# A two-layer fp32 feed-forward chain: the second layer's first product by Strassen's scheme

## The reference

```python
# 1: retention, 4 batches, 8 heads, 768 tokens, head size 64
state = gamma * state + k_t v_t^T;  y_t = scale * q_t state
# 2: first feed-forward, 512 -> 1024 -> 512
h = x @ w_in;  solu = h * softmax(h);  x = layernorm(solu) * g_ln @ w_out
# 3: second feed-forward, 512 -> 2048 -> 512
h = x @ w_in
g = h * np.cos(h)
out = g @ w_out
```

## Time and profile before

| | us |
|---|---|
| median of 3 executions | 1001.17 |
| lowest, highest | 1001.01, 1001.72 |
| span of the profiled execution | 1000.7 |
| PE busy | 961.5 (96%) |
| DVE busy | 714.2 (71%) |
| ACT busy | 430.6 (43%) |
| POOL busy | 259.8 (26%) |

### The profile page before, as it was taken

How to read it: one execution, slowest core, us unless ns; L and a number is a source line. 1 busy time by engine, 2 the same in 40 slices (tenths; PEclk the granted TensorE clock), 3 DMA queues, 4 the chain that set the end, 5 groups by cost and what they waited for, 6 DMA issues and landing times.

```text
span 1000.7 us, 13925 instructions
## 1 busy us (share of the span) xinstructions
PE 961.5 (96%) x4800; PEld 808.4 (81%) x4800; DVE 714.2 (71%) x1133; ACT 430.6 (43%) x786; POOL 259.8 (26%) x237
## 2 busy tenths in 40 slices
PE   2799999999999999999999999999999999999997
PEld 2688788888888888887788888888888888888886
DVE  6988788887888788885896566565665656656564
ACT  4645445445445454444554434333343433333333
POOL 5453454444544534512233002001100200110000
PEclk8899999999999999999999999999999999999999
DMA  7411221311312212032352100010110101001001
GB/s 261 132 63 53 84 76 53 106 52 52 105 52 64 94 52 88 28 95 87 104 168 64 43 1 26 17 42 0 42 42 0 41 0 42 0 0 42 1 1 43
DMA packets 39857, 57.92 MB, mean 58 GB/s; under 512 B 3217, under 2 KB 15505, under 8 KB 39825
## 3 DMA queue, kind: packets, MB, share of 16 engines
q1 hardware_dynamic: 39824, 57.50, 17.9%
HBM read 44.90 MB, written 12.58 MB: 57 GB/s over the span
## 4 chain that ended last, share of the span: by engine, by line
PE 77%; DVE 14%; issue 4%; ACT 3%; DMA 0%; POOL 0%; SPq 0%; DVEq 0%; ACTq 0%; POOLq 0%
PE bank L284 26%; PE bank L286 25%; PE bank L285 25%; DVE p_l L800 4%; DVE z_l L879 2%; DVE nmax L844 2%; ACT z_h L622 2%; DVE p_m L793 1%; DVE x_l L824 1%; PE bank L484 1%; ACT p_h L589 1%; DVE w1o_l L838 1%; DVE w1i_l L833 1%; DVE stats L855 1%; DVE work L849 0%
## 5 line engine op out<-in xcount | busy, mean ns | idle before, releaser
L908 DVE SCALAR_TENSOR_TENSOR red<-turns,bank 128x512 f32<-128x512 int32 x96 | 65.8, 686 | 155.2 <-ACT turns L648 155.2
L284 PE MATMUL bank<-w2o_h,g_h 128*128 128x512 f32 x384 | 149.8, 390 | 1.3 <-DVE g_l L926 1.2
L284 PE MATMUL bank<-y_g,w2i_h 128*128 (+1 forms) x384 | 149.6, 390 | 0.0
L286 PE MATMUL bank<-w2o_h,g_l 128*128 128x512 f32 x384 | 149.4, 389 | 0.0
L286 PE MATMUL bank<-y_g,w2i_l 128*128 (+1 forms) x384 | 149.4, 389 | 0.0
L285 PE MATMUL bank<-y_g,w2i_h 128*128 (+1 forms) x384 | 149.4, 389 | 0.0
L285 PE MATMUL bank<-w2o_l,g_h 128*128 128x512 f32 x384 | 149.4, 389 | 0.0
L648 ACT ACTIVATE turns<-bank 128x512 int32<-128x512 f32 x96 | 57.3, 597 | 202.5 <-PE bank L286 202.5
L714 POOL TENSOR_TENSOR y_g<-y_raw,y_g 128x512 f32 (+1 forms) x24 | 31.9, 1333 | 307.6 <-ACT y_g L643 307.6
L654 ACT ACTIVATE gg<-red 128x512 f32<-128x512 f32 x96 | 60.7, 632 | 91.5 <-DVE red L912 91.5
L284 PEld LDWEIGHTS bank<-w2o_h,g_h 128*128 128x128 f32 x384 | 72.1, 188 | 17.5 <-issue 2.7
(11 more groups left out here) (96 smaller groups left out, 2061.9 us busy)
## 6 DMA issues: line engine op xcount, KB each, us to landing
raw<-kT SPq DMA_DIRECT2D x24, 256.0 KB, 2.6
raw<-qT SPq DMA_DIRECT2D x24, 256.0 KB, 3.0
raw<-kn SPq DMA_DIRECT2D x24, 256.0 KB, 3.6
raw<-vn SPq DMA_DIRECT2D x24, 256.0 KB, 4.1
y_scratch<-work SPq DMA_DIRECT2D x24, 256.0 KB, 4.0
y_raw<-y_scratch SPq DMA_DIRECT2D x6, 1024.0 KB, 5.2
out<-o SPq DMA_DIRECT2D x24, 256.0 KB, 2.2
w_raw<-w_in SPq DMA_DIRECT2D x16, 256.0 KB, 2.8
```

The source lines that it names most:

```text
L284: eng.matmul(dst, ah, bh, start=first and i == 0, stop=False)
L286: m = eng.matmul(dst, al, bh, start=False, stop=last_one and i == n - 1)
L908: dve.scalar_tensor_tensor(red[:, f % 2, :], turns[:, f % 2, :], -TWO_PI_HI, ps_h2[:, f % 4, :], ALU.mult, ALU.add)\
```

## The change

The first half stays but for its tail. In the second half tokens go in 4 superblocks (`NS`) of 768, two halves of 384, and a superblock in 8 periods (`NJ`), each of two feature tiles, j (called LO) and j + 8 (HI). Feature halves, halves of the 512-long contraction and token halves make a 2 by 2 by 2 block product, which Strassen's scheme (in Winograd's form) does with seven products P1, P2, P6, P5, P3, P7, P4 in that order; each is 2 slices of the contraction by 3 matmuls of 384 columns. Their sums are taken so:

- weights: four sums `S1` to `S4` on POOL (`w2_in_sums`), then seven operands of 128 x 256 are split into high (ACT `w2_in_hi`) and low (DVE `w2_in_lo`), 1792 numbers a partition at once, once a period in superblock 0; they are stored to memory (`w2_split`) and loaded from there in superblocks 1 to 3, into a ring of two periods;
- tokens: four sums on POOL (`y_sums`, `y_sum4`), seven operands of 768 numbers split by ACT `y_hi` and DVE `y_lo` at places in period 7 and period 0 (`SPLIT_HI`, `SPLIT_LO`); DVE has the low parts now, POOL had them;
- results: two PSUM banks, `ps_x` and `ps_y2`, in which later products are added onto earlier ones; ACT copies three states (`e_1`, `e_2`, `e_5`) and one result (`c21`) out, DVE makes the three others (`c11`, `c12`, `c22`), 384 columns each.

The gate works on 768 columns, of LO and HI one after the other in the same two queues. Its square goes from DVE to ACT; the factor -2 goes to the copy of the outputs, of which DVE now has every second one. The second products `l4` have 6 token tiles, and stand between the seven products by the table `FILL`: HI of the period before the last, LO of the last. `ps_out` has six banks. Each product waits for the copy that frees its bank (`l3`). In the tail of the first half, P1 to P7 of period 0 replace `L3` 0 to 3.

```diff
-BLK = 512
-NBLK = NTOK // BLK
+HALF = 384
+SUPER = 2 * HALF
+NS = NTOK // SUPER
+NJ = NF // 2
+TS = SUPER // 128
...
+P1, P2, P6, P5, P3, P7, P4 = range(7)
+A21, A11, A12, A22, S1, S2, S3, S4 = range(8)
+WEIGHT = {P1: A11, P2: A12, P6: S2, P5: S1, P3: S4, P7: S3, P4: A22}
+LO, HI = 0, 1
+FILL = [[(HI, 0)], [(HI, 1), (HI, 2)], [(HI, 3)], [(HI, 4), (HI, 5)],
+        [(LO, 0), (LO, 1)], [(LO, 2), (LO, 3)], [(LO, 4), (LO, 5)]]
+SPLIT_HI = {(NJ - 1, P6): 0, (NJ - 1, P5): 1, (NJ - 1, P3): 2, (NJ - 1, P4): 3,
+            (0, P1): 4, (0, P2): 5, (0, P6): 6}
+SPLIT_LO = {(NJ - 1, P5): 0, (NJ - 1, P3): 1, (NJ - 1, P4): 2,
+            (0, P1): 3, (0, P2): 4, (0, P6): 5, (0, P5): 6}
...
+            def superblock(i, first, more):
+                for j in range(NJ):
+                    if first:
+                        store_split(j)
+                        if j + 2 < NJ:
+                            load_raw_in(j + 2)
+                        if j + 1 < NJ:
+                            load_raw_out(j + 1)
+                    if j + 2 < NJ:
+                        if not first:
+                            load_split(i, j + 2)
+                    elif more:
+                        load_split(i + 1, j + 2 - NJ)
+                    if j == 1 and not first:
+                        store_out(i - 1)
+                    if j == 2 and more:
+                        load_y(i + 1)
...
+            def l3(i, j, p):
+                if isinstance(i, int) and i == 0:
+                    pe.wait_ge(wi_lo, j + 1)
+                else:
+                    pe.wait_ge(ld_wc[p][j % 2], i * 64 + (16 * (j // 2 + 1) - 64))
+                if j == 0:
+                    block_wait(pe, yl_done, i, 7, p)
+                if p == P1:
+                    at(pe, c21_done, i, j - 1)
+                elif p == P2:
+                    at(pe, c12_done, i, j - 1)
+                elif p == P6:
+                    at(pe, e1_done, i, j)
+                elif p == P5:
+                    at(pe, c11_done, i, j)
+                elif p == P3:
+                    at(pe, e5_done, i, j)
+                elif p == P7:
+                    at(pe, e2_done, i, j)
+                else:
+                    at(pe, c22_done, i, j)
+                q = WEIGHT[p] - A11
+                dst = ps_y2 if p in (P2, P5, P3) else ps_x
+                products(pe, dst, [
+                    (ring[:, j % 2, q, 0, k, :], ring[:, j % 2, q, 1, k, :],
+                     yc_h[:, p, k, :], yc_l[:, p, k, :]) for k in range(2)],
+                    p in (P1, P2, P5), True, True).then_inc(p_done[p], 1)
+            def l4(i, j, r, t):
+                f = j + NJ * r
+                if t == 0:
...
+            def fill(i, j, p, first):
+                for r, t in FILL[p]:
+                    before = j - 2 if r else j - 1
+                    if before >= 0:
+                        l4(i, before, r, t)
+                    elif not first:
+                        l4(i - 1, before + NJ, r, t)
+            def superblock(i, first):
+                for j in range(NJ):
+                    for p in range(7):
+                        if not (first and j == 0):
+                            l3(i, j, p)
+                        fill(i, j, p, first)
 
...
+            def w2_in_hi(j):
+                act.wait_ge(ws_done, j + 1)
+                if j < 2:
+                    act.wait_ge(o_done, 2 * NT)
+                else:
+                    act.wait_ge(p_done[P4], j - 1)
+                    act.wait_ge(wc_stored[j % 2], 16 * (j // 2))
+                act.copy(ring[:, j % 2, :, 0, :, :].rearrange("p a k m -> p a (k m)"),
+                         w_st[:, A11:, :, :].rearrange("p a k m -> p a (k m)")).then_inc(wi_hi, 1)
+            def w2_out_hi(j):
+                act.wait_ge(ld_wo, 16 * (j + 1))
+                if j == 0:
+                    act.wait_ge(y_stored, 16 * NT)
+                act.copy(w2o_h[:, j:NF:NJ, :], wo_st[:, :, :]).then_inc(wo_hi, 1)
...
+            def slot(i, j, p, first):
+                if p == P1:
+                    before(turn, i, j, HI, first)
+                    at(act, p_done[P1], i, j)
+                    at(act, c11_done, i, j - 1)
+                    act.copy(e_1[:, :], ps_x).then_inc(e1_done, 1)
+                    before(g_hi, i, j, LO, first)
+                elif p == P2:
+                    before(sine, i, j, HI, first)
+                    if j == 1 and not first:
+                        out_copy(i - 1, 0)
+                elif p == P6:
+                    at(act, p_done[P6], i, j)
+                    at(act, c12_done, i, j - 1)
+                    act.copy(e_2[:, :], ps_x).then_inc(e2_done, 1)
+                    before(square, i, j, HI, first)
+                    if first and 0 < j < NJ - 1:
+                        w2_in_hi(j + 1)
+                    if first and j == 1:
+                        w2_out_hi(0)
+                elif p == P5:
+                    at(act, p_done[P5], i, j)
+                    at(act, c22_done, i, j - 1)
+                    act.copy(e_5[:, :], ps_y2).then_inc(e5_done, 1)
+                    before(g_hi, i, j, HI, first)
+                    if j == 1 and not first:
+                        out_copy(i - 1, 2)
+                    if first and j > 0:
+                        w2_out_hi(j)
+                elif p == P3:
+                    turn(i, j, LO)
+                    if j == 1 and not first:
+                        out_copy(i - 1, 4)
+                elif p == P7:
+                    sine(i, j, LO)
+                else:
+                    at(act, p_done[P4], i, j)
+                    if j > 0 or not first:
+                        at(act, g_done[HI], i, j - 1)
+                    act.copy(c_32[:, HI, 0, :], ps_x).then_inc(c21_done, 1)
+                    square(i, j, LO)
+                if (j, p) in SPLIT_HI:
+                    if j:
+                        if not isinstance(i, int) or i < NS - 1:
+                            y_hi(i + 1, SPLIT_HI[j, p])
+                    elif not first:
+                        y_hi(i, SPLIT_HI[j, p])
...
+            def w2_in_sums(j):
+                def w(a):
+                    return flat(w_st[:, a, :, :])
+                pool.wait_ge(ld_ws, 32 * (j + 1))
+                if j > 0:
+                    pool.wait_ge(wi_lo, j)
+                combine(w(S1), w(A21), w(A22), ALU.add).then_inc(s1_done, 1)
+                combine(w(S3), w(A11), w(A21), ALU.subtract)
+                pool.wait_ge(s1_done, j + 1)
+                combine(w(S2), w(S1), w(A11), ALU.subtract).then_inc(s2_done, 1)
+                pool.wait_ge(s2_done, j + 1)
+                combine(w(S4), w(A12), w(S2), ALU.subtract).then_inc(ws_done, 1)
+            def y_sums(i):
+                pool.wait_ge(ld_y, i * 16 + 16)
+                if isinstance(i, int) and i == 0:
+                    pool.wait_ge(q_lo[1], NT)
+                    pool.wait_ge(n_lo, NT)
+                else:
+                    block_wait(pool, yl_done, i, 7, P7 - 7)
+                combine(t_3, b22, b12, ALU.subtract).then_inc(t3_done, 1)
+                block_wait(pool, t3_done, i, 1, 0)
+                combine(t_1, b12, b11, ALU.subtract).then_inc(t1_done, 1)
+                block_wait(pool, t1_done, i, 1, 0)
+                combine(t_2, b22, t_1, ALU.subtract).then_inc(t2_done, 1)
+            def y_sum4(i):
+                block_wait(pool, yl_done, i, 7, P2)
+                block_wait(pool, t2_done, i, 1, 0)
+                combine(t_4, b21, t_2, ALU.subtract).then_inc(t4_done, 1)
+            def w2_out_lo(j):
+                pool.wait_ge(wo_hi, j + 1)
+                subtract(w2o_l[:, j:NF:NJ, :], wo_st[:, :, :], w2o_h[:, j:NF:NJ, :])\
+                    .then_inc(wo_lo, 1)
...
+            def w2_in_lo(j):
+                dve.wait_ge(wi_hi, j + 1)
+                parts = ring[:, j % 2, :, :, :, :].rearrange("p a h k m -> p a h (k m)")
+                dve.tensor_tensor(parts[:, :, 1, :],
+                                  w_st[:, A11:, :, :].rearrange("p a k m -> p a (k m)"),
+                                  parts[:, :, 0, :].bitcast(F32), ALU.subtract).then_inc(wi_lo, 1)
...
+            def slot(i, j, p, first):
+                if p == P1:
+                    before(gate, i, j, LO, first)
+                    before(reduce, i, j, HI, first)
+                    before(g_lo, i, j, LO, first)
+                elif p == P2:
+                    at(dve, p_done[P2], i, j)
+                    at(dve, e1_done, i, j)
+                    dve.tensor_tensor(c_32[:, LO, 0, :], ps_y2, e_1[:, :], ALU.add)\
+                        .then_inc(c11_done, 1)
+                    before(reduce2, i, j, HI, first)
+                elif p == P6:
+                    before(gate, i, j, HI, first)
+                    if j == 1 and not first:
+                        out_copy(i - 1, 1)
+                elif p == P5:
+                    before(g_lo, i, j, HI, first)
```

(53 more changed lines are left out.)

510 lines of the change are left out of this document (256 added, 254 removed).

## The result

| | before | after |
|---|---|---|
| median, us | 1001.44 (4 executions, 1001.01 to 1001.85) | 1057.64 (4 executions, 1057.18 to 1059.04) |
| ratio after / before | | 1.056, 95% interval 1.055 to 1.058 |
| span of the profiled execution | 1000.7 | 1055.6 |

The change makes the kernel 56 us slower; 1038 was forecast, with a range of 1008 to 1062. Here are the head, the busy table, the chain and two DMA rows of the page of the kernel after; the first two answer to the earlier trace rows.

The account below looks back on a forecast made before the run. PE bounds the kernel, paying by columns. 484.8 to period 1, 22.8, 97.0 and 22.5 for superblock 0, 370.6, 12.2, 13.9, 4 and clock 4.6 gave 1032.4; 5.0 of output and 0.5 made about 1038, range 1008 to 1062.

Parts of the forecast that it names:

- What PE gains: First products on PE: 1344 matmuls of 384 columns at 0.173 us replace 1152 at 0.227, gaining 28.6 us.
- 13.9 + 4: Superblocks 1 to 3: token splits and output copies add 13.9 us, POOL's token sums colliding with DVE add 4.
- Periods 2 to 6: Superblock 0's converting periods: 19.4 us each, 97.0 together; 99.3 with 2.3 of clock counted behind period 1.
- the reduction's +0.8: Periods 2 to 6: POOL's `w2_out` conversion holds up reduce LO by 0.8 us; its weight sums add 0.8 to the second reduction.
- count nothing (up to 12 if it grows): Periods 2 to 6: PE's wait near 2.5 us was given no clock loss, up to 12 us if it grows.
- The 2.3 us a fall: Periods 1 and 7: PE waits over 3.5 us, then runs slowly at about 2.3 us each, 4.6 together.
- The rival that let the clock fall in every converting period: Superblock 0: waits of 3 us or more bring five more slow restarts, periods at 20.6, total 1056; chance 0.2.
- Tail: End of the first half: 2 us for added token splits, then 19.05 us, so period 1 starts at 484.8.
- Period 1: Superblock 0: two `w2_out` conversions, the second load issued late, make it 22.8 us (bounds 17.8 and 26).
- The hiding rival (988): Conversions slide into idle time of ACT and DVE; superblock 0's periods 2 to 7 stay at 15.44, total 988; chance 0.13.
- if all else hid: Whole kernel: with only PE's gain counting and all other work hidden, the time would be near 972.
- SBUF rival (1017): POOL's work falls beside ACT's steps without SBUF collisions: periods 2 to 6 take 17.8 us, total 1017; chance 0.2.

Follow-up runs that it names:

- Experiment 5: Experiment 4's kernel with token splits and output copies of superblocks 1 to 3 moved into relay gaps and the fourth token sum on DVE: 1005.32 us.
- Experiment 7: Kernel after with only the tail of the first half reordered, including the next weight load issued ahead of the last tile's store: 1047.46 us.
- experiment 4: Kernel after with ACT's and DVE's weight splits moved later, low part of `w2_out` on DVE one period later, ACT's high part behind `g_hi` LO: 1023.14 us.
- experiments 3 to 5: Kernel after with weight splits moved (1037.68 us); then also `w2_out` low part on DVE (1023.14); then also token splits and output copies moved (1005.32).
- experiment 9: Kernel with all rearrangements (weights, `w2_out`, token splits, tail) plus one wait: POOL's token sums start after DVE's last low weight parts; 998.20 us.

## Why the prediction was right in its direction and 20 us low

The forecast's theory is borne out: PE gains its columns, and the relay of ACT and DVE in two strict queues, with conversions put between its steps and POOL colliding, costs more. It is the sizes that fell short, by 18.2 us of the span, and by 1.5 us between span and median (2.0 in the result, 0.5 taken).

- **What PE gains.** Starts of 384 columns were to be 0.173 apart; they are 0.173 singly (563.16, 563.33) and 0.177 on average, if the 512 keep 0.227: an undisturbed period takes 15.59, not 15.44, and PE gains 23.4 us instead of 28.6 (1344 at 0.177). That is 23 x 0.15 = 3.5 of the 3.7 us that the ordinary periods lack.
- **Token splits, output copies and sums in superblocks 1 to 3.** 13.9 + 4 were forecast; what stands over 24 x 15.59 is 22.2 in the trace. That period 7 and the next period 0 together are right to 0.1 us is luck: period 7 took 20.76 where 22.5 was forecast, period 0 took 22.01 where 20.1 was, with a second PE wait of 1.76 us (645.87) and the clock at 0.57 for 640 to 650. Experiment 5 got 17.2 back by moving the same work.
- **Periods 2 to 6.** 99.3 against 100.51 looks close, but is two errors that cancel. Without the clock's 1.57 a period is 18.53, not 19.4: the reduction's +0.8 came (0.72), the second one for the weight sums didn't (0.94 us at 558.87, before the sums began), 4.3 us less for five. And the clock, at which I "count nothing (up to 12 if it grows)", fell five times and cost 7.9, of which the 2.3 behind period 1 were counted: 5.6 more. The step that failed is that sentence. It took 3.0 us, the shorter of two idle times of the trace, for a limit, and waits of 2.08 to 2.11 us were followed by a fall all five times in this trace. The 2.3 us a fall was too much (1.57): of the "some 10 us" until the clock was back, a second wait of 3.59 us, which ended at 24.57 in the trace of before, was a part. The rival that let the clock fall in every converting period (0.2) had this right, though not by its condition, waits of 3 us or more. That its 1056 is nearest to the median of 1057.6 is partly luck: it holds nothing of the 8.0 in the tail and the 4.8 in period 1.
- **Tail.** 2 us for the added splits and 19.05 behind were forecast, and 8.0 more came. What I left out is that POOL's sums stand beside the last tile's `p_l`, and that the centring of the last tile stands in DVE's queue behind token splits that wait for ACT (1.28 us at 472.59, two splits ahead of it). Experiment 7 took back 7.4 of the 8.0.
- **Period 1.** The `w2_out` loads were seen, the weight load wasn't: SP issues it behind the last tile's store, which waits for the tail. +4.8; experiment 7 took back 3.9, experiment 4 took out the whole loss.
- **The hiding rival (988)** describes not this kernel but what it can become: conversions do hide in the gaps if they are put there (experiments 3 to 5), and with both changes the time is 998, 992 if POOL's token sums went too. What is left between 998 and the 972 of the forecast's "if all else hid" is, by the table of experiment 9, 4.9 us in periods 1 to 7 and 5.0 in superblocks 1 to 3, some 5 by the pace of 15.59; the remaining 10 or so lie outside the periods; I put them to the tail, but no run shows it.
- **SBUF rival (1017).** Its premise fell: the collisions are there. Removing POOL's low part gave 17 us by the medians and 12.0 by the two profiles, of which some 8 are the clock in periods 2 to 6; the 5 between them no trace shows.
